# A fused attention, expert and feed-forward kernel: y moves ahead of a reload, the second layer's first product inside the first layer's final tile, and a final store in three parts

## The reference

```python
# attention, batch 4, 8 heads, 768 steps, head size 48
for t in range(S):
    y[:, :, t] = einsum('bhd,bhde->bhe', q[:, :, t], state)
    v_old = einsum('bhde,bhd->bhe', state, kt)
    state = state + bt[:, :, :, None] * einsum('bhd,bhe->bhde', kt, vt - v_old)
# first layer, E = 8, D = 384, F = 1024; P from x @ w_gate, exp, 8 Sinkhorn rounds
for e in range(E):
    out += P[:, e:e + 1] * (maximum(x @ w1[e], 0.0) @ w2[e])
# second layer, 2048 wide
h = x @ w_in
out = (h * cos(h)) @ w_out
```

## Time and profile before

| what | value |
|---|---|
| median of 3 runs | 2314.76 us (2314.4 to 2317.61) |
| the profiled execution | 2311.99 us |
| its span, first to last instruction | 2310.2 us |
| mean granted TensorE clock | 0.977 |
| PE / PE loads / DVE / ACT / POOL busy | 96% / 80% / 44% / 32% / 30% |

### The profile page before, as it was taken

One profiled execution on the slowest core, in us unless ns is written; L12 is line 12 of the kernel. 1 busy time (PEld: TensorE's weight loads), 2 busy tenths in 40 slices (PEclk: granted clock), 3 DMA queues, 4 the chain that ended last, 5 costly groups with the idle time before them and its releaser, 6 DMA issues.

```text
span 2310.2 us, 40688 instructions
## 1 busy us (share of the span) xinstructions
PE 2217.6 (96%) x15460; PEld 1839.5 (80%) x15460; DVE 1005.3 (44%) x1621; ACT 744.4 (32%) x1288; POOL 689.5 (30%) x504
## 2 busy tenths in 40 slices
PE   3699998999999999999999999999999999999998
PEld 2688886788888888888888888888888877888887
DVE  4877752543222323232322322232323246777676
ACT  5555643211111111111111111111111126666665
POOL 3100001004533323232323233332323244444433
PEclk6689999999999999999999999999999999999999
DMA  5243332202111010111111111111111100000001
GB/s 159 65 125 98 100 88 90 86 22 58 41 28 32 27 46 28 31 30 29 31 41 32 27 32 27 43 29 32 28 31 27 45 23 14 14 14 14 0 14 68
DMA packets 85221, 102.35 MB, mean 44 GB/s; under 512 B 8384, under 2 KB 70144, under 8 KB 85120
## 3 DMA queue, kind: packets, MB, share of 16 engines
q1 hardware_dynamic: 85120, 100.91, 15.7%
HBM read 87.40 MB, written 8.75 MB: 42 GB/s over the span
## 4 chain that ended last, share of the span: by engine, by line
PE 74%; issue 12%; POOL 7%; DVE 5%; ACT 2%; SPq 1%; POOLq 0%; DMA 0%; DVEq 0%; ACTq 0%
PE p_h L597 5%; PE h L597 5%; PE h L599 5%; PE p_h L599 5%; PE p_h L598 5%; PE h L598 5%; POOL hlo L1104 5%; PE am_y L628 4%; PE am_y L627 4%; PE am_y L626 4%; PE chain_y L626 2%; PE chain_y L627 2%; PE chain_y L628 2%; PE o_y L626 2%; PE o_y L627 2%
## 5 line engine op out<-in xcount | busy, mean ns | idle before, releaser
L1083 POOL TENSOR_TENSOR acc<-acc,py 128x512 f32 (+1 forms) x252 | 325.1, 1319 | 743.1 <-DVE py L1387 743.1
L947 ACT ACTIVATE hhi<-h 128x512 fp32r<-128x512 f32 x182 | 109.0, 599 | 771.4 <-PE h L599 771.4
L1354 DVE SCALAR_TENSOR_TENSOR hlo<-h,hhi 128x512 fp32r<-128x512 f32 x182 | 125.9, 692 | 475.8 <-ACT hhi L947 475.8
L1354 DVE SCALAR_TENSOR_TENSOR hlo<-p_h,hhi 128x512 fp32r<-128x512 f32 x182 | 125.8, 691 | 406.0 <-ACT hhi L947 406.0
L1051 POOL TENSOR_TENSOR wlo<-stage,whi (+1 forms) x114 | 156.4, 1374 | 438.2 <-ACT whi L837 413.3
L597 PE MATMUL h<-xhi,whi 128*128 (+1 forms) x690 | 269.8, 391 | 2.9 <-DVE scr L1455 2.9
L597 PE MATMUL p_h<-xhi,whi 128*128 (+1 forms) x690 | 269.2, 390 | 0.1
L598 PE MATMUL h<-xlo,whi 128*128 (+1 forms) x690 | 269.1, 390 | 0.0
L599 PE MATMUL h<-xhi,wlo 128*128 (+1 forms) x690 | 268.9, 390 | 0.0
L599 PE MATMUL p_h<-xhi,wlo 128*128 (+1 forms) x690 | 268.5, 389 | 0.0
L598 PE MATMUL p_h<-xlo,whi 128*128 (+1 forms) x690 | 268.5, 389 | 0.0
(11 more groups left out here) (223 smaller groups left out, 4066.7 us busy)
## 6 DMA issues: line engine op xcount, KB each, us to landing
stage<-wcat SPq DMA_DIRECT2D x40, 768.0 KB, 4.3
pb<-p_scratch SPq DMA_DIRECT2D x84, 256.0 KB, 4.7
kq<-kqt SPq DMA_DIRECT2D x48, 192.0 KB, 3.4
kn<-krow SPq DMA_DIRECT2D x6, 768.0 KB, 5.1
kT<-kta SPq DMA_DIRECT2D x24, 192.0 KB, 4.8
v<-vrow SPq DMA_DIRECT2D x24, 192.0 KB, 4.7
kb<-krow SPq DMA_DIRECT2D x24, 192.0 KB, 5.0
out<-acc SPq DMA_DIRECT2D x6, 768.0 KB, 3.8
```

The source lines that it names most:

```text
L947: act.activation(hhi[:, j, :], hps[j % 2][:, 0:TILE], ACT.Relu).then_inc(s["hhi_done"], 1)
L1083: pool.tensor_tensor(y, y, py[:, d, :], ALU.add).then_inc(s["added"], 1)
L1354: dve.scalar_tensor_tensor(out=hlo[:, j, :], in0=hps[j % 2][:, 0:TILE], scalar=0.0, in1=hhi[:, j, :].bitcast(F32), op0=ALU.max, op1=ALU.su ...
```

## The change

Four places differ.

1. SP: `reload(0)` is taken out of the loop and stands behind the last 20 y moves.
2. The second layer's first up product (`up2(0, 0, 0, 0)`) stands on PE inside the first layer's final tile, between mm2(2) and mm2(3). DVE splits tile 3 in the final tile behind its third `hlo`, reduces the first argument ahead of that tile's `py` products, and makes the first gate ahead of the last of them. Tiles 4 and 5 are split in six pieces of one feature chunk (128x512), one behind the Sin of steps 0, 1, 2, 4, 5 and 6 on ACT, and one behind the next step's gate on DVE.
3. In the last two steps of the last pass DVE makes the low parts, not POOL.
4. The last tile is stored in three DMAs of 256 KB, one for each feature chunk, each with its own wait.

To make room for these, loops of the last expert and the last pass are written out on PE, DVE and POOL.

```diff
+X2_AT = (0, 1, 2, 4, 5, 6)
+X2_PARTS = [(t, d) for t in (NT - 2, NT - 1) for d in range(DC)]
...
-                if c == 2 and g == NG - 1:
-                    reload(0)
                 if c % 2 == 1:
                     move_y(i // 2)
+        reload(0)
         store_early(EARLY - 1)
...
-        with sp.Fori(0, NT) as t:
+        with sp.Fori(0, NT - 1) as t:
             sp.wait_ge(s["y2_evac"], ((PASSES2 - 1) * NT + t) * DC + DC + 6)
             sp.dma_start(out[:, :, bass.ds(t * TILE, TILE)], x_of(t)).then_inc(s["stored"], 16)
-        sp.wait_ge(s["stored"], 16 * NT)
+        for d in range(DC):
+            sp.wait_ge(s["y2_evac"], (PASSES2 * NT - 1) * DC + d + 1 + 6)
+            sp.dma_start(out[:, d, (NT - 1) * TILE:], x_part(NT - 1, d)).then_inc(s["stored"], 16)
+        sp.wait_ge(s["stored"], 16 * (NT - 1 + DC))
...
+        def up2(tile, buf, j, g):
+            pe.wait_ge(s["g_done"], g + 1)
+            if j == 0:
+                pe.wait_ge(s["x2_done"], tile + 1)
+            up(tile, buf, j, j % 2).then_inc(s["mm1b"], 1)
+        def tile(e, half, tp, k, mode, final=False):
...
             mm2(2)
+            if final:
+                pe.wait_ge(s["wlo_done"], PASSES1 * NT + NT // 2)
+                up2(0, 0, 0, 0)
             mm2(3)
...
+        with pe.Fori(0, NT // 2) as tp:
+            for k in range(2):
+                tile(N_EXP - 1, 0, tp, k, WEIGHED)
+        with pe.Fori(0, NT // 2 - 1) as tp:
+            for k in range(2):
+                tile(N_EXP - 1, 1, tp, k, WEIGHED)
+        for k in range(2):
+            tile(N_EXP - 1, 1, NT // 2 - 1, k, WEIGHED, final=k == 1)
...
             if q == 0:
-                pe.wait_ge(s["wlo_done"], PASSES1 * NT + NT // 2)
-                up2(0, buf, 0, 0)
                 up2(0, buf, 1, 1)
...
+        def x2_hi_part(t, d):
+            act.wait_ge(s["added"], (PASSES1 * NT - NT + t) * DC + 2 * DC)
+            act.activation(xhi[:, t, d, :], x_part(t, d), ACT.Copy).then_inc(s["x2hi"], 1)
...
                 act.activation(rr[:, j % 2, :], rr[:, j % 2, :], ACT.Sin, scale=-1.0,
                                bias=halfpi[:, 0:1]).then_inc(s["cos_done"], 1)
+                if first and st in X2_AT:
+                    x2_hi_part(*X2_PARTS[X2_AT.index(st)])
...
             if q == 0:
                 steps(0, 0, True)
-                for t in range(NT - 2, NT):
-                    x2_hi(t)
             with act.Fori(1 if q == 0 else 0, NT // 2) as tp:
                 steps(q, tp, False)
...
+        for q in range(PASSES2 - 1):
             with pool.Fori(0, NT // 2) as tp:
                 for st in range(2 * CH):
...
+                    split_h2(q, tp, st)
+                    if st in SPLITS:
                         split_lo((q + 1) % 2, tp * 2 + SPLITS.index(st), PASSES1 + q + 1)
+        with pool.Fori(0, NT // 2 - 1) as tp:
+            for st in range(2 * CH):
+                split_h2(PASSES2 - 1, tp, st)
+        for st in range(2 * CH - 2):
+            split_h2(PASSES2 - 1, NT // 2 - 1, st)
...
-        def tile(e, half, tp, k, mode):
...
                                          op1=ALU.subtract).then_inc(s["h_split"], 1)
+                if after_third and j == 2:
+                    after_third()
...
+            if before_y:
+                before_y()
             for d in range(DC):
+                if before_last and d == DC - 1:
+                    before_last()
                 dve.wait_ge(s["y_done"], g * DC + d + 1 + 3)
                 y = yps[k][d][:, 0:TILE]
...
-        with dve.Fori(1, NT // 2) as tp:
-            for k in range(2):
-                tile(N_EXP - 1, 1, tp, k, WEIGHED)
-                x2_lo(tp * 2 + k - 2)
+        for k in range(2):
+            tile(N_EXP - 1, 1, 1, k, WEIGHED)
+            x2_lo(k)
+        tile(N_EXP - 1, 1, 2, 0, WEIGHED)
+        x2_lo(2)
...
+        def reduced(j, g):
...
+            dve.wait_ge(s["k_done"], g + 1)
+            dve.scalar_tensor_tensor(out=r, in0=kint[:, j % 2, :], scalar=-C1, in1=hp, op0=ALU.mult,
+                                     op1=ALU.add).then_inc(s["r1_done"], 1)
+            dve.wait_ge(s["r1_done"], g + 1)
+            dve.scalar_tensor_tensor(out=r, in0=kint[:, j % 2, :], scalar=-C2, in1=r, op0=ALU.mult,
+                                     op1=ALU.add).then_inc(s["r_done"], 1)
...
+        def gated(j, g):
+            dve.wait_ge(s["cos_done"], g + 1)
...
+            dve.wait_ge(s["h2_split"], g + 1)
+            dve.tensor_tensor(gg[:, j % 2, :], hps[j % 2][:, 0:TILE], rr[:, j % 2, :], ALU.mult).then_inc(s["g_done"], 1)
...
+        def x2_lo_part(t, d, n):
+            dve.wait_ge(s["x2hi"], NT - 2 + n)
+            ins = dve.tensor_tensor(xlo[:, t, d, :], x_part(t, d), xhi[:, t, d, :].bitcast(F32), ALU.subtract)
+            if d == DC - 1:
+                ins.then_inc(s["x2_done"], 1)
+        def split_h2(j, g):
+            dve.wait_ge(s["hhi2_done"], g + 1)
+            dve.wait_ge(s["h2_split"], g + 2)
+            dve.tensor_tensor(hlo[:, j, :], gg[:, j % 2, :], hhi[:, j, :].bitcast(F32), ALU.subtract).then_inc(s["h2_split"], 1)
+        def steps(q, tp, prev, first=False, last=False):
             for st in range(2 * CH):
                 j = st % CH
...
+                if not (first and st == 0):
+                    reduced(j, g)
+                if last and st == 2 * CH - 1:
+                    split_h2(j - 1, g - 1)
                 if prev and 2 <= st < 5:
                     take(*prev, 1, st - 2)
...
                 if st == 7:
                     take(q, tp * 2, 0, 1)
                     take(q, tp * 2, 0, 2)
...
+                if not (first and st == 0):
+                    gated(j, g)
+                if first and st > 0 and st - 1 in X2_AT:
+                    n = X2_AT.index(st - 1)
+                    x2_lo_part(*X2_PARTS[n], n + 1)
+                if last and st == 2 * CH - 1:
+                    split_h2(j, g)
...
+        tile(N_EXP - 1, 1, 2, 1, WEIGHED, before_y=lambda: reduced(0, 0), before_last=lambda: gated(0, 0), after_third=lambda: x2_lo(3))
         for q in range(PASSES2):
-            steps(q, 0, (q - 1, NT - 1) if q else None)
-            if q == 0:
-                for t in range(NT - 2, NT):
-                    x2_lo(t)
-            with dve.Fori(1, NT // 2) as tp:
-                steps(q, tp, (q, tp * 2 - 1))
+            steps(q, 0, (q - 1, NT - 1) if q else None, first=q == 0)
+            if q < PASSES2 - 1:
+                with dve.Fori(1, NT // 2) as tp:
+                    steps(q, tp, (q, tp * 2 - 1))
+            else:
+                with dve.Fori(1, NT // 2 - 1) as tp:
+                    steps(q, tp, (q, tp * 2 - 1))
+                steps(q, NT // 2 - 1, (q, NT - 3), last=True)
         for t in range(DC):
             take(PASSES2 - 1, NT - 1, 1, t)
```

More of the change, by code:

```diff
@@ L676, in _ @@
                 tile(1, 1, tp, k, WEIGHED)
-        with pe.Fori(2, N_EXP) as e:
+        with pe.Fori(2, N_EXP - 1) as e:
             for half in range(2):
@@ L681, in _ @@
                         tile(e, half, tp, k, WEIGHED)
-        def up2(tile, buf, j, g):
-            pe.wait_ge(s["g_done"], g + 1)
-            if j == 0:
-                pe.wait_ge(s["x2_done"], tile + 1)
-            up(tile, buf, j, j % 2).then_inc(s["mm1b"], 1)
+        with pe.Fori(0, NT // 2) as tp:
[6 more added lines that the diff above has]
+            tile(N_EXP - 1, 1, NT // 2 - 1, k, WEIGHED, final=k == 1)
         def down2(tile_in_pair, buf, j, g, tile_no):
@@ L1098, in _, with split_h2 @@
                         tile(e, half, tp, k, WEIGHED)
-        for q in range(PASSES2):
+        def split_h2(q, tp, st):
+            j = st % CH
+            pool.wait_ge(s["hhi2_done"], (q * NT + tp * 2) * CH + st + 1)
+            pool.tensor_tensor(hlo[:, j, :], gg[:, j % 2, :], hhi[:, j, :].bitcast(F32),
+                               ALU.subtract).then_inc(s["h2_split"], 1)
+        for q in range(PASSES2 - 1):
             with pool.Fori(0, NT // 2) as tp:
                 for st in range(2 * CH):
-                    j = st % CH
-                    pool.wait_ge(s["hhi2_done"], (q * NT + tp * 2) * CH + st + 1)
-                    pool.tensor_tensor(hlo[:, j, :], gg[:, j % 2, :], hhi[:, j, :].bitcast(F32),
-                                       ALU.subtract).then_inc(s["h2_split"], 1)
-                    if q < PASSES2 - 1 and st in SPLITS:
-                        split_lo((q + 1) % 2, tp * 2 + SPLITS.index(st), PASSES1 + q + 1)
+                    split_h2(q, tp, st)
+                    if st in SPLITS:
+                        split_lo((q + 1) % 2, tp * 2 + SPLITS.index(st), PASSES1 + q + 1)
+        with pool.Fori(0, NT // 2 - 1) as tp:
[3 more added lines that the diff above has]
+            split_h2(PASSES2 - 1, NT // 2 - 1, st)
     @block.vector
@@ L1336, in columns, with tile @@
                               ALU.mult).then_inc(s["sunk"], 1)
-        def tile(e, half, tp, k, mode):
```

(34 more changed lines are left out.)

## The result

The kernel after takes 2309.23 us, median of 11 runs (2305.27 to 2312.57), and the kernel before 2314.4 us beside it (11 runs, 2310.59 to 2319.22). The ratio is 0.9971, with a 95% interval of 0.9961 to 0.9980, so between 4.6 and 9.0 us are gone. The forecast was 4.74 us less, 2310.0 us.

The account below looks back on a forecast made before the run. PE, busy for 96% of the span, was taken as the bound, so only its waits, low clock and tail could change. 2.76 + 0.33 + 1.65 = 4.74 us off 2314.76 gave 2310.0 us, range 2304.5 to 2312.9.

Parts of the forecast that it names:

- Part 1: End of attention: y moves ahead of the reload let PE's gate product start 2.76 us earlier, from 0 to 4.5.
- it brings nothing: Rival at the end of attention: moves land late or another wait ends there; 2312.8 us, chance 0.18.
- Part 2: Boundary of the layers: removed PE waits mostly come back in small ones; gain 0.3 us, from -0.5 to some 7.5.
- gate 9: Second layer: this gate comes at 1945.0, against 1945.29 before; behind it both kernels run alike.
- pace the steps at 4.86 us: Second layer's early steps: 4.86 us for each of five periods behind gate 1, against PE's need of 4.08 us.
- the pieces hide: Rival at the boundary: ACT and DVE don't pace the steps, part 2 is worth about 5.5 us; 2304.8 us, chance 0.15.
- gate 1 escapes: Rival at the boundary: DVE's chunk 1 reduction beats POOL's third add, gate 1 comes 1.06 us earlier; 2309.0 us, chance 0.19.
- the clock falls in the paced steps: Rival in the second layer: at 1.2 GHz PE's matmuls take some 7.5 us a step, five steps cost 13 us; 2323, chance 0.03.
- lower bound of -0.5: Boundary of the layers: -0.5 us if the clock falls in the new 2.0 us wait and the next product comes late.
- Part 3: End of the kernel: low parts on DVE give 0.3 us and the split store 1.36; 1.65 us, 0.8 to 2.2.
- one third is left: Last store: two thirds go while DVE still adds, so only a third remains, 1.36 us less.
- The thirds queue up: Last store: the lower bound of its saving, 0.8 us, if the three DMAs queue.

Follow-up runs that it names:

- e10: Kernel of e9, with ACT making the last attention tile's high part ahead of its third eviction; 2298.41 us, ratio to before 0.9919.
- e5: Kernel after, with POOL making only 32 of 512 columns of the low parts in the second layer's first eight steps; chunk 1 to chunk 11 took 41.92 us.
- e8: Kernel after, with POOL's first low part of the second layer ahead of the final tile's last add; ratio 0.9986.
- e1: Kernel before, with only the reload of tile 0 put behind the last 20 y moves; 2313.47 us, ratio 0.9997.
- e3: Kernel before, with only the last tile's store split into three DMAs; ratio 1.0000, last take to end of span 2.46 us.
- e4: Kernel after, with the last tile in one DMA of 768 KB with a constant address; last take to end of span 4.20 us.
- e6: Kernel after, without the twelve split pieces of tiles 4 and 5, low parts whole; chunk 1 to chunk 11 took 42.22 us.
- e11: Kernel after, with POOL making the last two low parts again; chunk 1 to the last take took 405.48 us.
- e2: Kernel before, with only the boundary of the layers changed; ratio 1.0000, chunk 1 to chunk 11 took 46.81 us.
- e7: Kernel after, with the split pieces moved, ACT's ahead of Abs and DVE's ahead of the gate; 2303.94 us, ratio to before 0.9952.
- e9: Kernel after, with the edits of e7 and e8 together; 2301.81 us, ratio 0.9939.
- e12: Kernel after, with only ACT's split pieces moved ahead of Abs, DVE's left behind the gate; chunk 1 to chunk 11 took 44.52 us.

## Why the prediction was right, and where not

**What bounds.** PE's stream takes as long after as before, 1494.1 us from the gate product to chunk 1. Between the traces this distance differs by 2.7 us, and it follows the granted clock behind the gate product. Its mean over the 10 us from there is

| traces | clock | to chunk 1 |
|---|---|---|
| e10 | 1.00 | 1492.70 |
| e5, e8 | 0.85 to 0.86 | 1493.65 to 1493.90 |
| before, after, e1, e3, e4, e6, e11 | 0.80 to 0.84 | 1494.08 to 1494.53 |
| e2, e7, e9, e12 | 0.71 | 1494.97 to 1495.40 |

What moved lies in waits of PE that the list named, in the clock behind them, and behind PE's last matmul.

**Part 1, 2.76 us.** Measured 2.91 (e1: 2.90), so the rival that it brings nothing is out. The moves started where the argument put them, ACT's evictions were late next, and the wait that stayed is 3.85 us against the 4.0 forecast. Of the 0.15 us between the two, 0.10 is that `xhi` starts before the last eviction has ended. The clock fell all the same, in the kernel after at 408.4, 0.3 us behind the start of the gate product. Where it doesn't, in e10, 1.5 us come on top, against the 1.7 that I gave it as a bound.

**Part 2, 0.33 us.** Measured between +0.2 and -0.5 us, by the traces: 46.98 before (46.49 in e1) against 46.81 in three traces and 47.46 in one. The gates came as forecast, gate 9 at 44.79 in e4 for 44.66. But the term that this was taken from, the kernel before, is only one case of it. In e1 the same code had no low clock behind its wait of 2.44 us and reached chunk 11 0.5 us earlier, and against that the change loses 0.3 us. So part 2 gained nothing that can be relied on, and that the sum came out near the median is in part luck: with e1 and e4 as the traces, part 2 came 0.6 us below its forecast and part 3 0.6 us above. The step that carries it, that ACT, DVE and the reduction's wait for POOL pace the steps at 4.86 us, is shown by e5, e6 and e7; each of the five periods measured 4.85 to 4.87, but for the one of 5.48 with the low clock. PE had five waits for the gate of 0.28 to 0.56 us, not some seven of 0.7. The rival that the pieces hide is out for this order of the code, and right for another: against before e7 gives 4.7 us by it, near the 5.5 that it was priced at, and e9, which also takes away the wait for the first low part, 5.9. The rival that gate 1 escapes is out too: for chunk 1 L1443's counterpart took 1.69 to 1.75 us in all eleven traces with the new boundary, and for chunks 2 to 7 it took 1.47 to 1.69 in the order of the kernel after. The rival that the clock falls in the paced steps didn't come in the form that it was given: in one trace of eleven it fell, and one step took 5.48 us, not five steps 7.5 each. The new wait for the first low part was 1.8 us, not 2.0, and the clock fell behind it in one of the seven traces that have it with 1.73 to 1.78 us ahead of this product (the kernel after; not e2, e4, e6, e7, e11 and e12). That case costs 0.65 us (47.46 against 46.81), more than the 0.4 that I gave it, and with it part 2 is at its lower bound of -0.5.

**Part 3, 1.65 us.** Two terms. The low parts on DVE gave 0.4 us in eight of nine traces (e11 against e4), for 0.3 forecast, and nothing in the profile of the kernel after. The store gave 1.87, above the bound of 1.6. The failed step is "one third is left": when the last take ends only 0.6 of some 2.2 us of data have moved. The thirds queue up, which I had priced at only 0.8 us, and what is saved is that the first starts 1.39 us earlier and another 0.5 us sooner behind its take. My sum had nearly the same figure, 1.36, by another way, which is luck, and left the 0.5 out.

**The sum.** 4.74 us forecast. The profiles of before and after give 4.2 us by the distances. With the traces of after's code whose clock stays up it is 2.9 + 0.2 + 0.4 + 1.9 = 5.4 us, and 4.9 if the boundary is taken against e1 (-0.3). The medians are 5.2 apart, and the interval of the ratio is 4.6 to 9.0 us. That the change is faster by over 0.2%, to which I gave 0.6, holds by the ratio, but only just: the interval's end is at the bound of 0.2% (0.9980). What lies between 5.4 us and the ratio's centre of 6.7 isn't explained by any run; the spread of the attention stage is large enough for it.

**Left open.** Why the attention stage takes 381.9 to 390.7 us in traces of the same code. The granted clock differs there: its mean from 100 to 150 us is lowest, 0.66 to 0.69, in three of the traces with the longest stage (e7, e2 and e12, `yT` at 388.84 to 390.65). But the kernel before, e8 and the kernel after all had 0.83, with 383.40, 384.24 and 388.22, so this isn't all of it. Nor was it tried why the distance from chunk 11 to the last take is half a microsecond shorter in e6, e7, e9 and e10 (357.5 to 357.6) than in e4 and e8 (358.15).

## What to carry to other kernels

When work is moved into a chain of engines, look for the place where the engine that takes it idles anyway, not for a step where its busy share is low: the same twelve pieces cost 4.5 us between Sin and the next rounding, and 0.1 us ahead of Abs and of the gate (e7 against e6). Where DVE and POOL share a step, order the streams so that DVE's two-input SBUF instruction starts first, or that the one which meets POOL is off the chain. And measure one part by a distance between two fixed instructions of the trace: here it told 0.1 us where eleven runs of the whole told 3. Take the distance short, and look at the granted clock inside it: over long stretches the same code differed by 0.5 us and more.

## What the runs showed of the hardware

A reduction on DVE with two SBUF inputs (0.69 us alone) that starts within a POOL instruction of about 1.3 us (a low part or a weight split) ends 0.54 to 0.55 us behind it, in all 582 cases of the second layer in the fourteen traces, and takes 1.35 to 1.82 us, by how far in it starts; next to a POOL instruction of 0.25 us it stays at 0.69 (e5). The other way round POOL pays: where DVE starts first, POOL's instruction takes 1.63 to 1.84 us. A store of 256 KB is issued in 0.36 us and its data starts 0.8 us behind the instruction that it waits for; for 768 KB it is 0.57 and 1.35 us. Behind the same wait of 1.8 us the granted clock fell in one execution and not in six others, and behind one of 2.44 us in two (before, e3) and not in a third (e1).
